# Attention, top-1 experts and a dense MLP on one core: router inputs loaded after the first rotation, the last tail's logits by matrix products, w2 of the first expert in free row tiles, nested conditions for the last expert tiles

## The reference

```python
# attention: B, H, S, Dh = 4, 8, 576, 64
q_rot, k_rot = rotate(q), rotate(k)             # cos, sin tables over positions
attn = softmax(q_rot @ k_rot.T / 8)             # minus the row's maximum, + 1e-9 in the sum
x = (attn @ v).transpose(0, 2, 1, 3).reshape(2304, 512)
# top-1 mixture: E, F = 8, 1024
logits = normalised(x) @ normalised(expert_emb).T / tau
e = argmax(logits); gate = softmax(logits)[e]
x = gate * (relu(x @ w1[e]) @ w2[e])
# dense: 512 -> 2048 -> 512
h = x @ w_in
out = (h - tanh(h)) @ w_out
```

## Time and profile before

| | |
|---|---|
| runs | 1098.59, 1100.88, 1102.58 us, median 1100.88 us |
| profiled execution | 1100.7 us, span 1098.9 us |
| TensorE busy | 990.3 us, 90% of the span |
| VectorE, ScalarE, GpSimd busy | 54%, 53%, 39% |
| mean granted TensorE clock | 0.974 of full speed |

### The profile page before, as it was taken

One profiled execution on the slowest core, in us unless ns is written; L12 is line 12 of the kernel. 1 busy time (PEld: TensorE's weight loads), 2 busy tenths in 40 slices (PEclk: granted clock), 3 DMA queues, 4 the chain that ended last, 5 costly groups with the idle time before them and its releaser, 6 DMA issues. The chain is left out here.

```text
span 1098.9 us, 18622 instructions
## 1 busy us (share of the span) xinstructions
PE 990.3 (90%) x5620; PEld 876.7 (80%) x5621; DVE 596.5 (54%) x1194; ACT 581.4 (53%) x1275; POOL 424.8 (39%) x226
## 2 busy tenths in 40 slices
PE   0899999999997479999999747999999999999996
PEld 0799999898996358888888636878988898898895
DVE  4577777777775731111111105776666666666664
ACT  1577777777776442222222214666566556655653
POOL 1998878788710289169857023000000000000000
PEclk9999999999999599999999888999999999999999
DMA  7667666565832484324421024211000000000001
GB/s 207 188 183 205 176 162 163 172 180 170 271 72 73 145 312 138 77 78 141 147 69 57 21 89 132 64 43 49 1 29 0 0 29 0 29 0 0 29 1 29
DMA packets 58387, 108.02 MB, mean 98 GB/s; under 512 B 19424, under 2 KB 25056, under 8 KB 56032
## 3 DMA queue, kind: packets, MB, share of 16 engines
q1 hardware_dynamic: 49296, 89.98, 27.9%
q0 software_dynamic: 3440, 11.27, 3.4%
q10 hardware_dynamic: 5600, 6.08, 1.6%
HBM read 61.89 MB, written 17.03 MB: 72 GB/s over the span
## 5 line engine op out<-in xcount | busy, mean ns | idle before, releaser
L1552 PE MATMUL hd_ps<-y_hi,w_hi 128*128 128x384 f32 x384 | 132.2, 344 | 12.1 <-DVE g_sb L1721 11.9
L1552 PE MATMUL hd_ps<-y_lo,w_hi 128*128 128x384 f32 x384 | 130.1, 339 | 0.0
L1552 PE MATMUL hd_ps<-y_hi,w_lo 128*128 128x384 f32 x384 | 130.0, 339 | 0.0
L1621 ACT ACTIVATE mag<-hd_ps 128x384 f32<-128x384 f32 x96 | 47.2, 492 | 156.4 <-PE hd_ps L1552 145.9
L956 DVE TENSOR_REDUCE neg_max<-ps 128x1 f32<-128x576 f32 x144 | 108.1, 750 | 29.9 <-PE ps L545 27.4
L972 DVE TENSOR_TENSOR pt_lo<-ps,pt_hi 128x512 fp32r<-128x512 f32 x144 | 99.2, 689 | 44.4 <-ACT pt_hi L731 42.8
L731 ACT ACTIVATE pt_hi<-ps 128x512 fp32r<-128x512 f32 x144 | 86.8, 604 | 58.4 <-PE ps L592 57.1
L1570 PE MATMUL o_ps<-w_hi,g_hi 128*128 128x512 f32 x288 | 114.7, 398 | 2.2 <-DVE g_lo L1730 2.2
L1730 DVE TENSOR_TENSOR g_lo<-g_sb,g_hi 128x384 fp32r<-128x384 f32 x96 | 53.6, 558 | 113.5 <-ACT g_hi L1636 113.5
L1570 PE MATMUL o_ps<-w_lo,g_hi 128*128 128x512 f32 x288 | 114.2, 397 | 0.0
L1570 PE MATMUL o_ps<-w_hi,g_lo 128*128 128x512 f32 x288 | 113.7, 395 | 0.0
(11 more groups left out here) (216 smaller groups left out, 2438.6 us busy)
## 6 DMA issues: line engine op xcount, KB each, us to landing
w_stage<-in_w SPq DMA_DIRECT2D x32, 512.0 KB, 5.4
raw_qk<-in_qk SPq DMA_DIRECT2D x14, 1152.0 KB, 5.3
k_hh<-qk_hi SPq DMA_DIRECT2D x64, 144.0 KB, 2.6
k_ll<-qk_lo SPq DMA_DIRECT2D x64, 144.0 KB, 2.7
y_rows<-y_row ACTq DMA_DIRECT2D x20, 256.0 KB, 2.1
q_st<-qk_hi SPq DMA_DIRECT2D x32, 144.0 KB, 2.9
q_st<-qk_lo SPq DMA_DIRECT2D x32, 144.0 KB, 2.8
raw_v<-in_v SPq DMA_DIRECT2D x32, 128.0 KB, 2.2
```

Of the source, the lines that this page charges most:

```text
L1552: op = nc.tensor.matmul(hd_ps[f % 2][:, 0:G], w[:, c, cols], y[:, c, :], start=c == 0 and h == 0, stop=c == DC - 1 and h == 2)
```

## The change

Four edits.

1. *Start.* ScalarE's queue issues the cos and sin tables first, then the embeddings and tau. The router's `table` and `token` go behind the third load of raw q and k on SP, the identity, the fold matrix and the embeddings for it (six transfers, `consts_in`) from ScalarE's queue to SP's, behind `stack_k(0)`. `stack_q(0)` is issued by ScalarE, and a new semaphore `first_a` counts the stacks of pair 0's first head, so that its score units need those alone. On VectorE both rotations stand ahead of the norms of the embeddings; the newton chain stands between the fifth and the sixth maximum of pair 0.
2. *Last tail's logits.* They are not passed by DMA any more. The summed logits without the last pair's tail are made ahead; `tail_sb` is written first of the last pair's three results, two products with halves of the identity bring its logits to their rows in PSUM (`late_ps`), and an addition puts them in.
3. *First w2.* Its four chunks land in `token_rows` tiles 13 to 20 (`early_half`), issued by SP in the attention block once all rows are stored and squared, no longer in `w_stage` as it comes free in the expert block. `AHEAD` is 13: tiles 13 to 20 are gathered after the first set is split. ScalarE makes w2's high parts ahead of tile 0's h_hi, VectorE the low parts ahead of tile 0's h_lo; the exp of the gate moves behind them.
4. *Conditions.* Each of the seven conditions on TensorE now stands inside the one before it.

```diff
-AHEAD = HELD
+AHEAD = HELD - 8
+def early_half(rows, c):
+    at = HELD - 8 + (c - UP) * 2
+    return rows[:, at:at + 2, :]
...
             load_v(0)
-            sp.dma_start(sums[:, 0, :], a["tri"]).then_inc(route_in, 16)
-            sp.dma_start(table[:, 0:TABLE], a["table"].partition_broadcast(P)).then_inc(route_in, 16)
-            sp.dma_start(token[:], a["token"]).then_inc(route_in, 16)
+            sp.dma_start(sums[:, 0, :], a["tri"]).then_inc(tri_in, 16)
             sp.wait_ge(first_k_done, 1)
-            stack_k(0)
-            sp.wait_ge(rope_done, 1)
-            stack_q(0)
+            stack_k(0, (first_a, stack_in[0]))
+            sp.dma_start(id_sb[:], a["ident"]).then_inc(consts_in, 16)
+            sp.dma_start(fold_sb[:, :, E:E + DH], a["fold"].rearrange("p (g d) -> p g d", g=PB)).then_inc(consts_in, 16)
...
+            sp.wait_ge(tail_done, 1)
+            pass_tail(PAIRS - 1, 1, "rows", last_in)
             sp.wait_ge(x_done, PAIRS * 2)
-            pass_tail(PAIRS - 1, 1, "logits", last_logits)
             store_main(B - 1, late)
-            pass_tail(PAIRS - 1, 1, "rows", last_in)
...
             sp.wait_ge(x_stored, 16 * 2 * (B + 1))
-            sp.wait_ge(route_in, 16 * 3)
+            sp.wait_ge(sq_done, T)
+            for c in range(UP, CHUNKS):
+                sp.dma_start(early_half(rows, c), weight_chunk(a["w1"], a["w2"], expert, c)).then_inc(second_half[c - UP], 16)
+            sp.wait_ge(route_in, 16 * 2)
...
+            pe.wait_ge(tail_done, 1)
+            for u in range(2):
+                last = nc.tensor.matmul(late_ps, id_sb[:, u * TAIL:(u + 1) * TAIL],
+                                        tail_sb[1][:, u * (E + DH):u * (E + DH) + E], start=u == 0, stop=u == 1)
+            last.then_inc(late_ready, 1)
...
-            act.dma_start(emb_sb[:], a["emb_t"].rearrange("(c p) e -> p c e", p=P)).then_inc(emb_in, 16)
-            act.dma_start(tau_sb, a["tau"].partition_broadcast(P)).then_inc(emb_in, 16)
             act.dma_start(cos_sb[:, 1, :], a["cos"]).then_inc(tables_in, 16)
             act.dma_start(sin_sb[:, 1, :], a["sin"]).then_inc(tables_in, 16)
+            act.dma_start(emb_sb[:], a["emb_t"].rearrange("(c p) e -> p c e", p=P)).then_inc(emb_in, 16)
+            act.dma_start(tau_sb, a["tau"].partition_broadcast(P)).then_inc(tau_in, 16)
...
+            act.wait_ge(rope_done, 1)
+            for u in range(2):
+                for half, part in enumerate((hi, lo)):
+                    to = slice(half * DH, (half + 1) * DH)
+                    act.dma_start(q_st[0][u][to, u * TAIL:u * TAIL + S].bitcast(F32),
+                                  part[u * DH:(u + 1) * DH, 0, :].bitcast(F32)).then_inc((first_a, stack_in[0])[u], 16)
...
+            nc.vector.tensor_tensor(raw_l[:, :, last_main], raw_l[:, :, last_main],
+                                    lg_all[:, last_main, (H - 1) * E:H * E].rearrange("p t e -> p e t"), ALU.add)
+            dve.wait_ge(late_ready, 1)
+            chain(nc.vector.tensor_tensor(raw_l[late_rows, :, T - 1], raw_l[late_rows, :, T - 1], late_ps, ALU.add))
+            dve.wait_ge(route_in, 16 * 2)
             route()
...
-            expert = sp.value_load(plan[0:1, EXPERT, 0:1], min_val=0, max_val=E - 1)
-            for c in range(UP, CHUNKS):
-                sp.wait_ge(w_split, c - RING + 1)
-                sp.dma_start(staged(stage, c), weight_chunk(w1, w2, expert, c)).then_inc(w_landed[c % RING], 16)
...
+            def rest(t):
+                if t < MT - 2:
+                    with pe.If(fourth > t - 2):
+                        tile(t)
+                        rest(t + 1)
...
-            for t in range(T - 2, MT - 2):
-                with pe.If(fourth > t - 2):
-                    tile(t)
+            rest(T - 2)
...
+            for c in range(UP, CHUNKS):
+                act.wait_ge(second_half[c - UP], 16)
+                nc.scalar.activation(chunk_of(w_hi, slot, c).rearrange("p (k d) -> p k d", d=D), early_half(rows, c),
+                                     ACT.Identity).then_inc(first_hi, 1)
+            tile(0, start=True)
```

More of the change, by code:

```diff
@@ L99, in spots, with attention @@
     return put
-def attention(nc, a, first_x, w_at, free_at, rows, tail_dram, x_dram, y_dram, id_sb, stage, w_hi, w_lo, pos_i, plan, gid, raw_l,
+def attention(nc, a, first_x, second_half, w_at, free_at, rows, tail_dram, x_dram, y_dram, id_sb, stage, w_hi, w_lo, pos_i, plan, gid, raw_l,
               norm):
@@ L227, in attention @@
         route_in = sem("route_in")
+        tri_in = sem("tri_in")
+        tau_in = sem("tau_in")
         first_k_in = sem("first_k_in")
@@ L531, in scores @@
                 g = p * TILES + i
-                if i == 0:
-                    pe.wait_ge(stack_in[r], (half + 1) * STACKS)
+                if first and i == 0:
+                    pe.wait_ge(first_a, STACKS // 2)
+                if i == (MIX if first else 0):
+                    pe.wait_ge(stack_in[r], stacks_of(r, half + 1))
                 if not (first and i < 2):
@@ L1033, in _ @@
             nc.vector.tensor_tensor(by_sin[:], raw1[:, 2:4, :], sin_sb[:], ALU.mult).then_inc(mult_done, 1)
+            for i in range(TILES):
+                maximum(0, 0, i)
+                if i == MIX:
+                    dve.wait_ge(tau_in, 16)
+                    chain(nc.vector.reciprocal(inv_tau, tau_sb))
+                    dve.wait_ge(emb_root, 1)
+                    newton(chain, nc, emb_n[:, 2, :], emb_n[:, 1, :], emb_n[:, 0, :], emb_n[:, 3, :])
+                    chain(nc.vector.tensor_scalar(emb_n[:, 4, :], emb_n[:, 2, :], inv_tau, None, ALU.mult))
             dve.wait_ge(consts_in, 16 * 6)
@@ L1185, in _ @@
             last = pool.value_load(plan[0:1, LAST, 0:1], min_val=0, max_val=E - 1)
-            with pool.Fori(0, 1) as before:
+            for t in range(AHEAD, HELD):
+                gather(t)
+            with pool.Fori(0, 3) as before:
                 next_set(before)
-            for t in range(AHEAD, MT):
+            for t in range(HELD, MT):
                 gather(t)
-            with pool.Fori(1, E - 1) as before:
+            with pool.Fori(3, E - 1) as before:
                 next_set(before)
@@ L1315, in take_y, with tile @@
                 act.dma_start(y_dram[bass.ds(t * P, P), :], y_row[:]).then_inc(y_stored, 16)
-            def tile(t, start=False, second=False, turn=True, last=False, split=False):
+            def tile(t, start=False, second=False, turn=True, last=False):
                 for f in range(2):
@@ L1381, in split_w @@
             def split_w(c):
+                lo, hi, raw = chunk_of(w_lo, slot, c), chunk_of(w_hi, slot, c).bitcast(F32), stage[:, c % RING, :]
                 if c >= UP:
                     dve.wait_ge(first_hi, c - UP + 1)
-                nc.vector.tensor_tensor(chunk_of(w_lo, slot, c), stage[:, c % RING, :],
-                                        chunk_of(w_hi, slot, c).bitcast(F32), ALU.subtract).then_inc(w_split, 1)
+                    raw = early_half(rows, c)
+                    lo, hi = (w.rearrange("p (k d) -> p k d", d=D) for w in (lo, hi))
+                nc.vector.tensor_tensor(lo, raw, hi, ALU.subtract).then_inc(w_split, 1)
             count = [0]
@@ L1404, in _ @@
             take_x(1)
+            for c in range(UP, CHUNKS):
+                split_w(c)
             for t in range(2):
@@ L1407, in _ @@
                     low_h(t, f)
-                if t == 0:
-                    for c in range(UP, CHUNKS):
-                        split_w(c)
                 take_x(t + 2)
@@ L1786, in build @@
         first_x = ctx.enter_context(nc.semaphore("first_x"))
+        second_half = [ctx.enter_context(nc.semaphore(f"second_half{c}")) for c in range(UP)]
         with ExitStack() as inner:
```

98 lines of the change are left out of this document (54 added, 44 removed).

## The result

The changed kernel takes 1090.7 us (median of 7 runs, 1088.27 to 1094.53) against 1100.88 us of the kernel before beside it (7 runs, 1096.73 to 1105.13): ratio 0.9908, 95% interval 0.9879 to 0.9936. That is faster by 10.2 us, where 22.6 us were forecast, and outside the range. The profiled execution took 1088.51 us, 1.8 us more than its span.

What follows compares the result with a forecast made beforehand. TensorE is busy almost throughout; waits at the start, router, first expert tile and skip bound the rest. 8.0 + 2.8 + 3.0 + 8.8 = 22.6 us off 1100.7 gives 1078.1, 1078.3 against the median; range 1075 to 1087.

Steps and rivals of the forecast that it cites:

- Term A: Start: earlier tables and q stacks bring pair 1's scores from 42.87 to 34.9 us; 8.0 us won, between 6.1 and 8.5.
- so it is covered: Start: pair 0, newton chain included, is through at 33.7 us, before pair 1's stack at 34.9, so the chain costs nothing.
- Term B: Router: dropping the logits' DMA round trip and reduction for two additions and small products wins 2.8 us, between 2.1 and 3.4.
- I charge nothing, at worst 1 us: Expert block's start: first gather, beside four w2 transfers, has its rows in time, 4.5 us after issue.
- Term C: First expert tile: w2 landed early lets down(0) start at about 395.3 instead of 398.35 us; 3.0 us, between 1.5 and 3.1.
- Rival 3: First products with w2, down(0): TensorE's hesitation goes, 2.9 us more won, total 1075.4 us; chance 0.12.
- Term D: Skip after expert tile 17: one long condition instead of five false ones, 7.2 us, plus 1.6 us of clock; 8.8 us.
- the 108 ns for a compare-and-branch: Skip: by this figure the four conditions saved are 0.4 us and the nesting is worthless; the trace disagreed for three of five.
- Rival 1: Skip: the jump saves nothing, the sequencer draws every page between; gain there falls to 0.4 us, total 1086.7; chance 0.12.

Runs made afterwards that it cites:

- emb_late: Changed kernel with the embeddings' squares behind the rotation of q and the clamp behind pair 1's multiplications: 1088.71 us, ratio 0.9904.
- chain_in_psum: Changed kernel with the newton chain's results in unused PSUM columns instead of SBUF, same operations and place: 1081.8 us, ratio 0.984.
- dense_gathers_later: w2_in_block with GpSimd issuing the dense stage's gathers from tile 4 on only after ScalarE's first magnitude: 1072.65 us, ratio 0.9838.
- w2_in_block: Changed kernel with chain partly in PSUM, embeddings' squares and clamp later, w2's transfers issued by SP in the expert block after the first gather landed: 1079.37 us, ratio 0.9811.
- skip_undone: Changed kernel with the last expert tiles' conditions side by side again instead of nested: 1098.3 us (nine executions), ratio 0.9977.
- gathers_later: Kernel before, with only the gathers of tiles 13 to 20 moved behind the split of the first expert's weights: 1096.91 us, ratio 0.9959.

## Why the prediction was wrong, point by point

**Term A** is the step that failed: 8.0 us forecast, 0.5 lost. Two sentences of it were wrong, and one wait is missing from it.

The first gave "0.3 us for emb_sq and the clamp that now lie between its rotations". It priced the work and not the wait (and the clamp stands behind both rotations, at 17.27 us). emb_sb was put behind the tables on ScalarE's queue and landed at 13.5 us; the squares stood ahead of the rotation of q and held it for 3.73 us. Alone its undoing earned nothing (emb_late), because the second fault stood behind it.

The second said the newton chain costs "at most 1.6 us", "seven ops at the 0.23 us of its last", "so it is covered". The 0.23 us were measured at 13.63, before GpSimd had its first long operation. In its new place the chain runs beside GpSimd and took 7.3 us (30.45 to 37.78). chain_in_psum shows the cause, by taking the results and all but one input of each operation out of SBUF and leaving all else. The Trainium skill has this as a rule ("SBUF — State Buffer", Who interferes with whom): GpSimd reads and writes through VectorE's second pair of ports; a VectorE operation with two inputs in SBUF, or one in a two-port mode, as a scaling can be, shares that pair, and whoever is second waits for the whole instruction. The traces agree for VectorE, which was the second each time: the two-input operations (L91 with 1.57 and 2.55 us, L1080 with 0.69 and 2.02) and the scalings (2.54, 2.29) waited, the reciprocals and the maxima, which read PSUM, did not, and each wait ended with GpSimd's operation. The rule speaks against this change and should have stood among the rivals. The wait that is missing from the term is TensorE's for the scaled fold_sb, which needs the chain's result and so moved behind the maxima too. With the faults mended, pair 1's scores begin at 35.8 to 36.6 us in six of the seven traces and at 37.7 in dense_gathers_later (forecast 34.9), and the start is worth 6.7 to 7.2 us.

**Term B** was right: 2.8 us to the gather's issue. From the last product with fold_sb to the issue it is 19.3 us in all five traces without the edit and 16.4 to 16.5 in all eleven with it. "I charge nothing, at worst 1 us" for the four transfers beside the gather was wrong by its upper bound: 1.9 us. The row I leaned on, q_st's 2.8 us, is one of 144 KB from SBUF to SBUF, not a gather of 128 rows beside 2 MB of weights. The trace of the kernel before had the gather's own 3.8 us, and the block began 4.5 us behind the issue only because the plan ended then; so 0.3 us were to spare, and the 2.2 us that the gather grew by cost 1.9. w2_in_block gives 1.8 of it back.

**Term C** was 3.6 us at down(0) instead of 3.0, right in mechanism: TensorE goes from the transposes of tile 2 (393.84) straight to down(0) (394.20). Its size is less sure, for no experiment takes it back alone. From the first transposes of the block to down(0) it is 21.3 to 22.7 us in the five traces without the edit and 19.0 to 20.3 in the eleven with it; the 3.6 rest on the slowest of the five, and on the two faster chips the difference is 1.2 to 1.6 us. **Rival 3** came as well: the 2.9 us of hesitation went. That it would stay because "Many transfers run there" was a guess in the wrong direction; what it waits for still has no row, and on another chip it was not there to begin with.

**Term D** was right, mechanism and size: one condition of 3.35 us, no dry time, the upper level behind it, 8.1 us (8.8 forecast); 7.6 by skip_undone. The 0.7 us too much are not told apart further. Of what the prediction took from the Trainium skill, the 108 ns for a compare-and-branch ("Advanced Engine Details and Errata", Control Flow Timing) lie above the two short conditions (68 and 79 ns) and far below the long one. Rival 1, that the far jump costs as much as the walk, is not what this trace shows: one wait of 3.35 us stood for all that was jumped over. That agrees with the Trainium skill ("Runtime: NRT & Kernel Launch", Instruction fetch mechanics), by which a taken branch out of the loaded code waits for a fetch of its target.

**Not in the sum at all**: the dense stage, 3.1 us. I took its 440 us as a constant that moves along. It is not one: from its first transposes to the end it is 439.8 to 444.3 us, with 12 to 32 products at the lower level, over the nine traces with the same dense code on the slower chips, and 434.9 to 435.2 us with 8 to 10 over four on the faster ones. The clock is only a part of that. Between slower and faster chips the difference lies ahead of the first product with w_out, at 17.4 to 22.1 us of the stage against 13.0 to 13.5, and on the slower chips the longest stage (gathers_later, 444.3 us) has 24 such products and not the most. What decides how long the clock stays down there is not settled; that its length makes the difference between the two kernels is read from the products' spacing, not shown by an experiment.

By the terms: 8.0 forecast against -0.5 is 8.5 us, the gather 1.9, the dense stage 3.1, together 13.5 too much; C with rival 3 gave 3.5 more than forecast. D fell 0.7 short, and 0.3 lie in the stretches between. 22.6 - 13.5 + 3.5 - 0.7 + 0.3 = 12.2, the difference of the spans.

## What to carry to other kernels

When an operation is moved, its duration moves only if the company does not change: look up what GpSimd does at the new place, and put one operand of small VectorE operations in PSUM when it is busy there. A small operation moved ahead of a large one brings its own transfer's landing along; ask for that before counting its microseconds. An operation moved back takes along all that needs its result, here the scaling of fold_sb. A wait can hide in a duration: compare the ends of neighbouring engines' rows, not only the idle times. And the distance from an issue to its first user is not the transfer's time when another wait ends later.

## What was unexpected of the hardware

A VectorE operation on 128x8 elements took 2.5 us instead of 0.17 beside a GpSimd operation, without any idle time in its row. The same program differs by 1% from chip to chip (1090 against 1100 us), and between the two traces of the kernel before 2.8 us of it lie in down(0), where TensorE hesitates in one and not in the other, 1.3 us between the block's first transposes and down(0), and 4.2 us in the dense stage ahead of its first product with w_out. A gather of 128 rows landed 5.9 to 6.7 us after its issue in the seven traces with four transfers of 512 KB beside it, and after 3.4 to 3.8 us in the nine without.
